# Grouping the products of probabilities and values three by three in the TensorE order of a clustered attention kernel

## The chip, the cores and the metric

The kernel runs on one core of one Trainium2 chip. The metric is the device time of one execution in microseconds (us), as the median of three runs.

## What is computed

The kernel computes three layers. First comes attention in which each query sees only the keys of its own cluster (2 batches, 8 heads, 768 positions, 64 columns each, 16 clusters):

```
mask = q_assign[:, :, :, None] == k_assign[:, :, None, :]
scores = scale * np.matmul(q, k.transpose(0, 1, 3, 2))
scores = np.where(mask, scores, -1000000000.0)
scores = scores - np.max(scores, axis=-1, keepdims=True)
attn = np.exp(scores)
attn = attn / (np.sum(attn, axis=-1, keepdims=True) + 1e-09)
return np.matmul(attn, v).astype(np.float32)
```

Here `q_assign` and `k_assign` are the nearest of 16 centroids by cosine. Its output, as 1536 tokens of 512 columns, goes through a layer of 8 experts of which each token takes one (512 to 1024 to 512 columns), and that output through a gated layer, `(x @ w_a) * (x @ w_b) @ w_out`, with 1536 inner columns. Only the attention is touched by the change.

## The kernel before, in words

The 16 pairs of batch and head are called heads here. The attention is a software pipeline over rounds `r`: in round `r` TensorE works on four heads at once. Each engine has one instruction queue, worked strictly in the order in which the program wrote it, with semaphores between the engines; nothing reorders it. The order of TensorE's queue is written out by hand in the loop over `rounds[2:]` (from line 1260 on), one line for each step:

- `scores_t(r, j)`, six times (lines 1212 and 1214): the transposed scores of key tile `j` of head `r`, 128 keys by 768 queries in two halves. ScalarE turns them into probabilities (`exps`, line 601). There are three PSUM banks for these halves.
- `times_v(r, j)`, six times (line 1227): the product of the probabilities of key tile `j` with its values, four recorded matmuls for the two halves of the queries, added up in the bank `o_ps` over the six tiles. It waits for the exponentials of its tile; the first waits also until the sum of the head before has been taken out of the bank, and the last releases `o_full`.
- `masked_scores(n, t)`, six times, for head `n = r + 2` (line 1174): the masked scores of query tile `t`, in one pair of banks, `pair`. VectorE takes each row's maximum out of it (`row_max`, `neg_max`, line 863). There is one such pair, so tile `t` waits for the maximum of tile `t - 1` (`mx_done`).
- `unit0(n, 0)` to `unit0(n, 6)` for head `n = r + 3`: transposes of queries and keys (units 0 to 3, line 1144), products with the centroids (units 4 and 5, line 1148) and a transpose of the logits (unit 6, line 1152), and units 7 and 8 (lines 1157 and 1160) for head `r + 2`. They share one bank `t0`: every unit waits until the one before it was taken out by ScalarE or VectorE. Unit 0 waits for `has_key` (line 907), which frees the bank after unit 8 of the head before.
- `unit1(kind, n)`: `max` for head `r + 1`, and `sum`, `out`, `mean` for head `r - 1`. They share the bank `t1`. `sum` (line 1188) adds the probabilities of head `r - 1` over the keys; `out` (lines 1194 and 1195) turns the attention output and the denominators `den` of head `r - 1` and waits until VectorE has made `den` (line 834).

VectorE's order around this is: after unit 8 it makes `has_key` (907), `has_tmp` (909), `found` (913) and `lost` (914), then `den` (834), then one copy of unit 1, the maxima of tiles 0 to 2, the copies of `high_parts` (795 and 797, for head `r + 4`), the maxima of tiles 3 and 4, `one_hot` (873 to 880), and the maximum of tile 5.

GpSimd adds up the probabilities (`add_probs`, line 346): the add of tile 1 waits for `sum` of head `r - 1`, the add of tile 2 follows directly, and the adds of tiles 3, 4 and 5 come later in the round, with `fill_lost` and `low_parts` between them. In the last two rounds VectorE does these adds.

Round 0 has no `sum`, `out` and `mean`, and takes in the masked scores of head 1 between its steps. Rounds 13 to 15 have no units 0 to 6, rounds 14 and 15 no masked scores either; these two have transposes for the next layer (`turn_x`, line 1241) instead. Where `out` is named below as a place, its first matmul (line 1194) is meant.

Of the kernel before, what the change touches and what calls it, by code (L numbers as in the profile page):

```python
# [73 lines left out]
def build(nc, q, k, v, centroids, expert_emb, tau, w1, w2, w_a, w_b, w_out, consts, out):  # L74
# [5 lines left out]
    with whole:  # L80
# [221 lines left out]
        def made(r):  # L302
            return {-3: [0, 1], -2: [2], -1: []}.get(r, [r + 3] if 0 <= r < HEADS - 3 else [])

        def masked(r):
            return {-2: [0, 1], -1: []}.get(r, [r + 2] if 0 <= r < HEADS - 2 else [])
# [19 lines left out]
        def early_tile(r, place):  # L326
            return [NT - 3 * (HEADS - r) + place] if HEADS - 2 <= r < HEADS else []
# [9 lines left out]
        def valid(n):  # L337
            return 0 <= n < HEADS
# [780 lines left out]
        def _(pe):  # L1119
# [44 lines left out]
            def masked_scores(n, t):  # L1164
                u = n % 4
                if t == 0:
                    pe.wait_ge(ops_in[u], 64 * (n // 4 + 1))
                two = masked_in(n, t)
                if n == 0 and t >= 2:
                    pe.wait_ge(mx_done, t - 1)  # L1170
                elif n > 0:
                    pe.wait_ge(mx_done, 6 * n + t)
                for half in range(2):
                    last = pe.matmul(two[:, half, 0:HALF], qb[u][0:96, t * P:(t + 1) * P],  # L1174
                                     kc[u][0:96, half * HALF:(half + 1) * HALF], start=True, stop=True)
                last.then_inc(mx_full, 1)

            def unit1(kind, n):
                i = t1_index[kind, n]
                if i:  # L1180
                    pe.wait_ge(t1_free, i)
                if kind == "max":
                    pe.wait_ge(mx_done, 6 * n + 6)
                    last = pe.transpose(t1[0:NT, 0:P], neg_max[n % 2][:], ident)
                elif kind == "sum":
                    pe.wait_ge(psum_ready, n + 1)
                    for half in range(2):
                        last = pe.matmul(t1[half * 32:half * 32 + 32, 0:HALF], ones_f[:, 0:32],
                                         prob_sum[:, half * HALF:(half + 1) * HALF], start=True, stop=True)
                elif kind == "out":  # L1190
                    pe.wait_ge(o_taken, n + 1)
                    pe.wait_ge(t1_free, t1_index["sum", n] + 1)
                    for j in range(3):
                        pe.transpose(t1[:, j * P:(j + 1) * P], o_sb[:, j * P:(j + 1) * P], ident)
                        last = pe.transpose(t1[:, HALF + j * 33:HALF + (j + 1) * 33], den[0:33, j * P:(j + 1) * P],
                                            cst[0:33, 0:33])
                else:
                    pe.wait_ge(vsum_ready, n + 1)
                    last = pe.matmul(t1[:, 0:D], ones_f[:], v_sum[n % 2][:], start=True, stop=True)
                last.then_inc(t1_full, 1)  # L1200

            def scores_t(n, j):

                u = n % 4
                if j == 0:
                    pe.wait_ge(max_in[u], 16 * (n // 4 + 1))
                for half in range(2):
                    i = 12 * n + 2 * j + half
                    if i >= 3:
                        pe.wait_ge(exp_done, i - 2)  # L1210
                    cols = slice(half * HALF, (half + 1) * HALF)
                    pe.matmul(st[i % 3][:, 0:HALF], kd[u][:, j * P:(j + 1) * P], qa[u][:, cols],  # L1212
                              start=True, stop=False)
                    pe.matmul(st[i % 3][:, 0:HALF], kc[u][0:97, j * P:(j + 1) * P], qb[u][0:97, cols],  # L1214
                              start=False, stop=True).then_inc(st_full, 1)

            def times_v(n, j):
                u, s = n % 4, n % 2
                pe.wait_ge(exp_done, 12 * n + 2 * j + 2)
                if j == 0:  # L1220
                    pe.wait_ge(v_in[u], 16 * (n // 4 + 1))
                    if n == 0:
                        pe.wait_ge(second_free, 9)
                    if n >= 1:
                        pe.wait_ge(o_taken, n)
                for half in range(2):
                    last = pe.matmul(o_ps[half * D:(half + 1) * D, 0:HALF], v_in_sb[u][:, j, :],  # L1227
                                     prob[s][:, j, half * HALF:(half + 1) * HALF],
                                     start=(j == 0), stop=(j == NT - 1))
                if j == NT - 1:  # L1230
                    last.then_inc(o_full, 1)

            def turn_x(j, to):

                if j == 0:
                    pe.wait_ge(x_done, H)
                    pe.wait_ge(mx_done, 6 * HEADS)
                if j >= 2:
                    pe.wait_ge(xt_taken, j - 1)
                for kk in range(KD):  # L1240
                    last = pe.transpose(to[:, kk * P:(kk + 1) * P], x_tok[:, j, kk * P:(kk + 1) * P], ident)
                last.then_inc(xt_full, 1)

            def logits(c):

                pe.wait_ge(xt_taken, max(3 * c + 3, 5 if c == 0 else 0))
                if c == 3:
                    pe.wait_ge(o_taken, HEADS)
                for kk in range(KD):
                    last = pe.matmul(logits_in[c][0:E, 0:HALF], en_t[:, kk, :],  # L1250
                                     x_t[c // 2][:, kk, (c % 2) * HALF:(c % 2 + 1) * HALF],
                                     start=(kk == 0), stop=(kk == KD - 1))
                last.then_inc(lgt_full, 1)

            for r in rounds[2:]:
                s_, p4 = valid(r), valid(r - 1)
                if s_: scores_t(r, 0)
                if r == 0: masked_scores(1, 2)
                for n in masked(r)[:1]: unit0(n, 7)
                if s_: scores_t(r, 1)  # L1260
                if r == 0: masked_scores(1, 3)
                if valid(r + 1) and r != 0: unit1("max", r + 1)
                if r == -1:
                    masked_scores(1, 0)
                    masked_scores(1, 1)
                if s_: scores_t(r, 2)
                if r == 0: masked_scores(1, 4)
                if p4: unit1("sum", r - 1)
                for n in masked(r)[:1]: unit0(n, 8)
                if s_: times_v(r, 0)  # L1270
                for n in made(r): unit0(n, 0)
                if r == 0: masked_scores(1, 5)
                if s_: times_v(r, 1)
                for t in early_tile(r, 0): turn_x(t, pair[:, t % 2, :])
                for n in made(r): unit0(n, 1)
                for n in masked(r)[:1]: masked_scores(n, 0)
                if r == -2: unit0(1, 7)
                if p4: unit1("out", r - 1)
                if r == HEADS: logits(0)
                for n in made(r): unit0(n, 2)  # L1280
                if s_: scores_t(r, 3)
                for n in masked(r)[:1]: masked_scores(n, 1)
                if r == -2: unit0(1, 8)
                for t in early_tile(r, 1): turn_x(t, pair[:, t % 2, :])
                for n in made(r): unit0(n, 3)
                if p4: unit1("mean", r - 1)
                if r == HEADS: logits(1)
                if s_: scores_t(r, 4)
                for n in masked(r)[:1]: masked_scores(n, 2)
                if r == -3: centroids_turned()  # L1290
                for n in made(r): unit0(n, 4)
                if s_: times_v(r, 2)
                if r == 0: unit1("max", 1)
                for n in masked(r)[:1]: masked_scores(n, 3)
                for n in made(r): unit0(n, 5)
                if s_: times_v(r, 3)
                for n in masked(r)[:1]: masked_scores(n, 4)
                if s_: scores_t(r, 5)
                for n in made(r): unit0(n, 6)
                if s_: times_v(r, 4)  # L1300
                for t in early_tile(r, 2): turn_x(t, pair[:, t % 2, :])
                for n in masked(r)[:1]: masked_scores(n, 5)
                if s_: times_v(r, 5)


            pe.wait_ge(x_done, HEADS)
# [193 lines left out]
```

## Time and profile before

| | |
|---|---|
| time before, median of 3 runs | 1043.55 us (1041.11 to 1053.14) |
| span of the profiled execution | 1031.7 us |
| TensorE busy | 888.3 us, 86% of the span |
| VectorE busy | 540.5 us, 52% |
| ScalarE busy | 293.2 us, 28% |
| GpSimd busy | 345.1 us, 33% |
| mean granted clock of TensorE | 0.932 |

The profile is of one execution; it records each instruction with its start, its duration, its engine and the program's line, and what ended the idle time before it. The span goes from the first to the last instruction; the device time of a run holds some 12 us more. The granted clock is given as a share of 2.4 GHz: 1.00 is 2.4 GHz, 0.50 is 1.2 GHz.

### The profile page before, as it was taken

To read this page: it belongs to the slowest core of one execution; us is meant where nothing else is said; L and a number is where in the kernel's file an instruction comes from. 1 tells how busy PE (TensorE), PEld (TensorE's weight loads), DVE (VectorE), ACT (ScalarE), POOL (GpSimd) and SP (SyncE) were. 2 spreads that over 40 slices of the span, in tenths; PEclk is the share of its full clock that TensorE was granted. 3 is DMA by queue.
4 is the path that set the end of the run, shared out by engine and by line. 5 is a ranking of instruction groups with operands and counts; after the bars stand their busy time and mean duration, and the time that the engine had idled before them with its cause. 6 is when DMAs were issued, how large, how long until landed. Compare 5 with 4: busy or idle time off the path is not lost.

```text
span 1031.7 us, 11850 instructions
## 1 busy us (share of the span) xinstructions
PE 888.3 (86%) x4205; PEld 626.6 (61%) x4206; DVE 540.5 (52%) x663; ACT 293.2 (28%) x558; POOL 345.1 (33%) x195
## 2 busy tenths in 40 slices
PE   5899999899999994287897778876999999999998
PEld 2545555555555542165675566764888888888886
DVE  5678788887787647156644664462621321131111
ACT  3234333343333334032331233131321211121111
POOL 5145665556554423634412442142500100000000
PEclk9599999999899897599999999887999999999999
DMA  4212322223211204554245523552100200000001
GB/s 116 71 46 76 86 83 71 64 74 88 63 45 50 102 27 173 214 193 176 95 147 193 189 97 132 194 193 82 62 1 1 62 21 1 1 29 13 1 1 41
DMA packets 41105, 86.93 MB, mean 84 GB/s; under 512 B 4216, under 2 KB 10584, under 8 KB 41056
## 3 DMA queue, kind: packets, MB, share of 16 engines
q1 hardware_dynamic: 39136, 79.99, 23.7%
q0 software_dynamic: 1920, 6.29, 1.8%
q8 instruction: 30, 0.49, 0.2%
q14 instruction: 19, 0.16, 0.0%
HBM read 60.53 MB, written 17.83 MB: 76 GB/s over the span
## 4 chain that ended last, share of the span: by engine, by line
PE 68%; DVE 15%; issue 13%; ACT 2%; DMA 1%; DVEq 1%; ACTq 0%; SPq 0%; POOL 0%
PE bank L1427 7%; PE bank L1428 7%; PE bank L1429 7%; PE bank L1227 4%; PE pair L1174 4%; PE first_pair L1212 3%; DVE wt L978 3%; PE bank L1367 3%; PE bank L1369 2%; PE first_pair L1214 2%; PE bank L1368 2%; DVE has_tmp L909 2%; PE bank L1212 2%; PE bank L1144 2%; PE first_pair L1444 2%
## 5 line engine op out<-in xcount | busy, mean ns | idle before, releaser
L552 POOL TENSOR_TENSOR wt<-w_raw,wt 128x2048 fp32r<-128x2048 f32 x20 | 118.3, 5935 | 180.3 <-DVE wt L970 180.2
L1101 DVE TENSOR_TENSOR g_sb<-bank,a_sb 128x512 f32<-128x512 f32 x36 | 24.9, 691 | 195.0 <-PE bank L1429 195.0
L978 DVE TENSOR_TENSOR wt<-w_raw,wt 128x2048 fp32r<-128x2048 f32 x21 | 116.3, 5543 | 2.0 <-ACT wt L680 1.8
L1427 PE MATMUL bank<-x_hi,wt 128*128 128x512 f32 x288 | 114.9, 399 | 1.4 <-DVE x_lo L1072 1.4
L1428 PE MATMUL bank<-x_lo,wt 128*128 128x512 f32 x288 | 114.5, 398 | 0.0
L1429 PE MATMUL bank<-x_hi,wt 128*128 128x512 f32 x288 | 114.5, 398 | 0.0
L863 DVE TENSOR_REDUCE neg_max<-pair 128x1 f32<-128x768 f32 x93 | 88.5, 951 | 43.8 <-PE pair L1174 43.8
L346 POOL TENSOR_TENSOR prob_sum<-prob_sum,prob 128x768 f32<-128x768 f32 x56 | 102.5, 1831 | 10.4 <-ACT prob L601 8.4
L1367 PE MATMUL bank<-wt,ht_hi 128*128 128x512 f32 x128 | 59.0, 461 | 50.0 <-DVE ht_lo L1042 50.0
L601 ACT ACTIVATE prob<-first_pair 128x384 f32<-128x384 f32 x128 | 59.5, 486 | 83.8 <-PE first_pair L1214 51.6
L1227 PE MATMUL bank<-prob,v_sb 128*64 128x384 f32 x384 | 82.7, 514 | 0.0
L1174 PE MATMUL pair<-kc,qb 96*128 96x384 f32 x186 | 60.1, 408 | 6.5 <-DVE neg_max L863 5.9
L1427 PEld LDWEIGHTS bank<-x_hi,wt 128*128 128x128 f32 x288 | 54.6, 190 | 15.1 <-DVE x_lo L1072 1.8
L1042 DVE TENSOR_TENSOR ht_lo<-bank,ht_hi 128x512 fp32r<-128x512 f32 x32 | 21.9, 684 | 79.5 <-ACT ht_hi L705 79.5
L1429 PEld LDWEIGHTS bank<-x_hi,wt 128*128 128x128 f32 x288 | 54.5, 189 | 13.4
L1367 PEld LDWEIGHTS bank<-wt,ht_hi 128*128 128x128 f32 x128 | 26.3, 206 | 59.8 <-DVE ht_lo L1042 34.1
L1428 PEld LDWEIGHTS bank<-x_lo,wt 128*128 128x128 f32 x288 | 54.6, 190 | 13.2
L761 ACT ACTIVATE a_sb<-bank 128x512 f32<-128x512 f32 x36 | 21.5, 598 | 129.8 <-PE bank L1429 129.7
L1174 PEld LDWEIGHTS pair<-kc,qb 96*128 96x128 f32 x186 | 33.6, 213 | 36.7 <-DVE neg_max L863 25.9
L1358 PE MATMUL first_pair<-wt,xt_hi 128*128 128x512 f32 x128 | 53.6, 419 | 1.9 <-DVE xt_lo L1036 1.9
L1368 PE MATMUL bank<-wt,ht_hi 128*128 128x512 f32 x128 | 55.0, 430 | 0.0
L1369 PE MATMUL bank<-wt,ht_lo 128*128 128x512 f32 x128 | 55.0, 430 | 0.0
(213 smaller groups left out, 1752.3 us busy)
## 6 DMA issues: line engine op xcount, KB each, us to landing
w_raw<-in_moe_w_dram SPq DMA_DIRECT2D x32, 1024.0 KB, 5.8
x_slots<-zeros SPq DMA_DIRECT2D x10, 512.0 KB, 3.6
x_slot<-x_slots SPq DMA_DIRECT2D x18, 256.0 KB, 3.0
y_slots<-y_sb SPq DMA_DIRECT2D x16, 256.0 KB, 2.3
q_raw<-in_q_dram SPq DMA_DIRECT2D x16, 192.0 KB, 2.4
k_raw<-in_k_dram SPq DMA_DIRECT2D x16, 192.0 KB, 2.5
v_sb<-in_v_dram SPq DMA_DIRECT2D x16, 192.0 KB, 2.4
qb<-qa SPq DMA_DIRECT2D x16, 192.0 KB, 2.6
```

The source lines that it names most:

```text
L346: ins = eng.tensor_tensor(prob_sum[:], prob[s][:, 0, :] if j == 1 else prob_sum[:], prob[s][:, j, :], ALU.add)
L552: pool.tensor_tensor(wt[chunk][:, 1, :], w_raw[c][:], wt[chunk][:, 0, :].bitcast(F32), ALU.subtract).then_inc(w_lo[1], 1)
L863: dve.tensor_reduce(neg_max[n % 2][:, t:t + 1], masked_in(n, t)[:, :, 0:HALF], AX.XY, ALU.max, negate=True).then_inc(mx_done, 1)
L978: dve.tensor_tensor(wt[chunk][:, 1, :], w_raw[c][:], wt[chunk][:, 0, :].bitcast(F32), ALU.subtract).then_inc(w_lo[0], 1)
L1174: last = pe.matmul(two[:, half, 0:HALF], qb[u][0:96, t * P:(t + 1) * P], kc[u][0:96, half * HALF:(half + 1) * HALF], start=True, stop=True)
L1227: last = pe.matmul(o_ps[half * D:(half + 1) * D, 0:HALF], v_in_sb[u][:, j, :], prob[s][:, j, half * HALF:(half + 1) * HALF], start=(j == 0 ...
L1367: pe.matmul(bank[5][:, :], ht_hi[:, ff, :], w[0], start=(ff == 0), stop=False)
L1368: pe.matmul(bank[5][:, :], ht_hi[:, ff, :], w[1], start=False, stop=False)
L1369: last = pe.matmul(bank[5][:, :], ht_lo[:, ff, :], w[0], start=False, stop=(ff == FT - 1))
L1427: pe.matmul(to[:, :], w[0], x2_hi[:, kk, :], start=(kk == 0), stop=False)
L1428: pe.matmul(to[:, :], w[0], x2_lo[:, kk, :], start=False, stop=False)
L1429: last = pe.matmul(to[:, :], w[1], x2_hi[:, kk, :], start=False, stop=(kk == KD - 1))
```

## The change

Four of the six `times_v` of a round are moved in TensorE's order, so that tiles 0, 1 and 2 stand directly behind one another at the place where tile 2 stood (behind `unit0(n, 4)`), and tiles 3, 4 and 5 at the place where tile 5 stood, at the end of the round. No instruction is added or removed, and no other engine's order is touched.

```diff
@@ -1267,10 +1267,8 @@
                 if r == 0: masked_scores(1, 4)
                 if p4: unit1("sum", r - 1)
                 for n in masked(r)[:1]: unit0(n, 8)
-                if s_: times_v(r, 0)
                 for n in made(r): unit0(n, 0)
                 if r == 0: masked_scores(1, 5)
-                if s_: times_v(r, 1)
                 for t in early_tile(r, 0): turn_x(t, pair[:, t % 2, :])
                 for n in made(r): unit0(n, 1)
                 for n in masked(r)[:1]: masked_scores(n, 0)
@@ -1289,18 +1287,18 @@
                 for n in masked(r)[:1]: masked_scores(n, 2)
                 if r == -3: centroids_turned()
                 for n in made(r): unit0(n, 4)
-                if s_: times_v(r, 2)
+                if s_:
+                    for j in (0, 1, 2): times_v(r, j)
                 if r == 0: unit1("max", 1)
                 for n in masked(r)[:1]: masked_scores(n, 3)
                 for n in made(r): unit0(n, 5)
-                if s_: times_v(r, 3)
                 for n in masked(r)[:1]: masked_scores(n, 4)
                 if s_: scores_t(r, 5)
                 for n in made(r): unit0(n, 6)
-                if s_: times_v(r, 4)
                 for t in early_tile(r, 2): turn_x(t, pair[:, t % 2, :])
                 for n in masked(r)[:1]: masked_scores(n, 5)
-                if s_: times_v(r, 5)
+                if s_:
+                    for j in (3, 4, 5): times_v(r, j)
```

## Rows read from the trace of the kernel before

**Rows 1.** TensorE's waits in the attention: us in total, times, longest.
```profile
PE bank L1194 <- DVE den L834: 18.3, 14, 2.0
PE pair L1174 <- DVE neg_max L863: 4.0, 9, 0.6
```

**Rows 2.** TensorE's timeline, head 8, up to `out`: start us, duration us, instruction.
```profile
221.93 0.87 PE L1227 MATMUL bank<-prob,v_sb 128*64 128x384 f32 x4
222.72 0.55 PE L1144 MATMUL bank<-cst,q_split 128*128 128x128 f32 x3
223.20 0.87 PE L1227 MATMUL bank<-prob,v_sb 128*64 128x384 f32 x4
224.00 0.55 PE L1144 MATMUL bank<-cst,q_split 128*128 128x128 f32 x3
226.25 0.30 PE L1194 MATMUL bank<-cst,o_sb 128*128 128x128 f32 x1 [1.35 <-DVE den L834]
```

**Rows 3.** The timeline of GpSimd and VectorE in the same stretch.
```profile
221.91 1.82 POOL L346 TENSOR_TENSOR prob_sum<-prob 128x768 f32<-128x768 f32 x1 [3.54 <-PE bank L1188]
222.24 1.55 DVE L909 TENSOR_TENSOR has_tmp<-hot,has_key 128x96 bf16<-128x96 bf16 x1
223.81 1.81 POOL L346 TENSOR_TENSOR prob_sum<-prob_sum,prob 128x768 f32<-128x768 f32 x1
224.11 1.53 DVE L914 TENSOR_SCALAR lost<-found 128x6 f32<-128x6 f32 x1
225.56 0.54 DVE L834 TENSOR_SCALAR den<-bank 33x384 f32<-33x384 f32 x1
```

**Rows 4.** The tile `has_tmp`: duration ns min/median/max over all heads.
```profile
L909 DVE TENSOR_TENSOR has_tmp<-hot,has_key x16: 207/1548/1551, 26.8 to 333.8; 128x96 bf16<-128x96 bf16 x16
```

**Rows 5.** TensorE's timeline, head 8, from the third product to the next head.
```profile
231.48 0.87 PE L1227 MATMUL bank<-prob,v_sb 128*64 128x384 f32 x4
...
234.95 0.62 PE L1174 MATMUL pair<-kc,qb 96*128 96x384 f32 x2 [0.50 <-DVE neg_max L863]
235.41 0.34 PE L1212 MATMUL first_pair<-qa,kd 128*128 128x384 f32 x1
...
236.21 0.57 PE L1152 MATMUL bank<-cst,logit_sb 48*128 48x48 f32 x6
236.71 0.87 PE L1227 MATMUL bank<-prob,v_sb 128*64 128x384 f32 x4
237.50 0.62 PE L1174 MATMUL pair<-kc,qb 96*128 96x384 f32 x2
...
238.85 0.45 PE L1212 MATMUL first_pair<-qa,kd 128*128 128x384 f32 x1
```

**Rows 6.** VectorE's timeline in that stretch: a cast, the maximum of tile 4.
```profile
232.06 1.97 DVE L797 CAST k_split<-k_raw 128x384 fp32r<-128x384 f32 x1
...
235.61 0.96 DVE L863 TENSOR_REDUCE neg_max<-pair 128x1 f32<-128x768 f32 x1 [0.71 <-PE pair L1174]
```

**Rows 7.** TensorE's timeline, round 13: two products in a row, masked scores, `out`.
```profile
333.46 1.51 PE L1227 MATMUL bank<-prob,v_sb 128*64 128x384 f32 x8
335.19 0.62 PE L1174 MATMUL pair<-kc,qb 96*128 96x384 f32 x2 [0.22 <-DMA kc<-hot_t]
337.76 0.30 PE L1194 MATMUL bank<-cst,o_sb 128*128 128x128 f32 x1 [1.96 <-DVE den L834]
```

**Rows 8.** Windows: us, TensorE busy (instructions), granted clock, DMA share, GB/s.
```profile
71.48:333.46 261.98, 241.24 (x1336) 0.95 0.25 68
200.76:221.93 21.17, 19.24 (x115) 1.00 0.28 77
265.20:288.74 23.54, 22.09 (x114) 0.85 0.20 53
185.00:188.20 3.20, 3.20 (x14) 0.51 0.09 20
338.60:345.30 6.70, 6.70 (x22) 0.50 0.00 0
```

## The prediction, made before the kernel ran

> **What bounds the kernel.** TensorE is busy for 86% of the span, so I read its waits first. The reader is to see in them that a full TensorE queue does not make its order free: 14 times in the attention `out` waits for `den`, 18.3 us together, far more than the 4.0 us for row maxima [rows 1]. So I read one full head (round 8; the twelve rounds 1 to 12 have this pattern) on all engines, then the grouped products that the trace already has, and last the clock by head.
>
> Between the end of unit 8 (221.93) and `out` (226.25) lie 4.32 us. TensorE fills them with two products, units 0 and 1 and a masked score, and idles 1.35 us [rows 2]. What lasts 4.32 us is VectorE's chain `has_key`, `has_tmp`, `found`, `lost`, `den`. Two of its small operations are long for what they do: `has_tmp` takes 1.55 us from 222.24 and ends with GpSimd's add at 223.7, `lost` takes 1.53 us and ends with the second add at 225.6 [rows 3]. Where no add ran, `has_tmp` took 0.207 us [rows 4]. The first add is released by `sum`, which stands ahead of the moved products. Nothing in this chain hangs on products 0 and 1, so it will not get shorter when they leave.
>
> The Trainium skill (SBUF: State Buffer, section "SBUF: two separate sides") says why: VectorE and GpSimd share a port pair as an exclusive lock, and the later one blocks for the whole instruction. The trace agrees with 1.55 against 0.207 us. This speaks against the change, since it makes the place of `den` independent of how TensorE is filled.
>
> **Part 1: products 0 and 1 leave the cover.** They take 0.79 (221.93 to 222.72) and 0.80 us (223.20 to 224.00) [rows 2], 1.6 us a head that were free under VectorE's chain. They are now paid later, and the idle time ahead of `out` grows from 1.35 to about 2.95 us. Part of that will be seen earlier: unit 0 reaches its wait for `has_key`, and unit 1 its wait for ScalarE's copy of unit 0. Neither moves `out`, nor does the masked score's wait for the DMA of `hot_t`: round 13, which has no units 0 and 1, waits 0.22 us for it and then another 1.96 us for `den`, and its `out` starts 4.30 us after unit 8, as in the full head [rows 7].
>
> **Part 2: grouping.** Alone, a product costs 0.80 us. Two behind each other are recorded with 1.51 us, one with 0.87 [rows 2, 7], so a second or third one costs 0.64. A group of three is 0.80 + 2 x 0.64 = 2.08 us, and a head saves 4 x 0.16 = 0.64 us.
>
> **Part 3: from the third product to the next head.** Now this takes 238.85 - 231.48 = 7.37 us, and it holds 0.50 us of waiting for the maximum of tile 3 [rows 5]. That wait has VectorE's cast in front (1.97 us, 232.06 to 234.03) [rows 6]. After the change the group of three comes before masked score 3, so the cast is over; but then unit 5 alone stands between masked scores 3 and 4. The turn from one masked score to the next cannot be shorter than 0.66 (234.95 to 235.61) + 0.96 for the maximum + some 0.04 of signalling = 1.66 us [rows 5, 6]. The new stretch:
>
> group 2.08; masked score 3 to 4, 1.66; masked score 4, 0.46 (to 235.41); scores 0.80 (to 236.21); unit 6, 0.50 (to 236.71); masked score 5, 0.55 (237.50 to 238.85, less a product of 0.80); group 2.08. Sum 8.13 us, against 7.37: +0.76 a head [rows 5].
>
> Masked score 5 doesn't wait: 0.46 + 0.80 + 0.50 = 1.76 is over 1.66. Unit 7 of the next head needs `hot`; the last group gives it 2.08 us against 0.80 now, so no loss there. `o_full` and so the loads of values and the exponentials' buffers come at the same place, at the end of the round. SP's queue sees nothing new.
>
> By rounds: 1 to 11, 11 x 0.76 = 8.4. Round 12 has no cast, so its 0.50 us wait doesn't exist today: +0.76 + 0.50 = 1.3. Round 0 likewise +1.3, less about 0.3, because products 0 and 1 stand among waits for other engines there: 1.0. Round 13 has neither unit 5 nor unit 6 as cover: 2.08 + 1.66 + 1.66 + 0.55 + 2.08 = 8.03 after; today's parts at full clock are four products 3.2, three masked scores 1.6, scores 0.8 and some 0.25 of waiting, 5.85: +2.2. Rounds 14 and 15 have pairs today; each saves 2 x 0.16: -0.6. Sum: 8.4 + 1.3 + 1.0 + 2.2 - 0.6 = **+12.3 us at an unchanged clock**. Its bounds: the hand-over from the small transposes to a product may save up to another 0.2 us a head, so 9; if waits show up that I take as hidden (0.2 us a head), 15.
>
> **Part 4: the clock.** A head takes 21.17 us at a clock of 1.00, but the twelve heads from 71.48 to 333.46 take 261.98 us, 7.9 us more than 12 x 21.17 [rows 8]. Six of the twelve have a stretch at 0.50 (1.2 GHz), and so has round 13; each begins shortly behind the wait for `den`, in round 13 at 338.60, 0.84 us after `out` started [rows 7, 8]. Five of the six are as short as the one of 3.20 us shown; the sixth is about twice as long and makes its head 23.54 us, 2.4 more than a full one, so the other five cost (7.9 - 2.4)/5 = 1.1 us each [rows 8]. Round 13, whose waits ahead of `out` are the longest (0.22 + 1.96) [rows 7], has 6.70 us at 0.50 [rows 8]. After the change every one of 13 heads has such a gap, 2.95 us instead of 1.35. I expect a slow stretch in all of them. A short one costs 1.1 now where the 0.50 us wait of part 3 swallows some; that wait is gone, so 1.6. 13 x 1.6 = 20.8 us, less what is paid now, 7.9 + 2.4 = 10.3: **+10 us**. Bounds: nothing, if the falls stay as rare; 13 x 2.4 - 10.3 = +21, if all are long.
>
> [...]
>
> **The sum.** 12.3 + 10 = 22.3 us on the profiled span of 1031.7: 1054. The median of the runs is 1043.55, 11.9 above that span, so 1043.55 + 22.3 = 1065.9, said as **1066 us**.
>
> **Rivals.**
> - *No more slow stretches.* The idle time ahead of `out` is now split in three, with units 0 and 1 between, and the clock may hold as often as now. Then 1043.6 + 12.3 = 1056 us (1052 to 1059). Against it: round 13's long slow stretch.
> - *All slow stretches long.* For it: round 13 again. 1043.6 + 12.3 + 21 = 1077 us.
> - *Faster.* One mechanism: `den` comes earlier. If GpSimd's adds no longer fell together with `has_tmp` and `lost`, each would give back 1.55 - 0.21 = 1.34 us [rows 3, 4], 2.7 a head, all of it idle time now uncovered. It decides from 0.76 us a head on. With both gone, the 12 full heads come out at 0.76 - 2.68 = -1.9 us each, 23 in all, and with the rest of the sum and fewer slow stretches 1017 us. Against it: `sum` releases the first add and unit 8 releases `has_key`, and both keep their places.
> - *About even.* One of the two collisions goes: 0.76 - 1.34 = -0.6 us a head, 7 in all, which the other rounds (+2.2, +1.0, +1.3) and some slow stretches make up: 1044 us.
>
> **How the numbers follow.** Forecast 0.55, no more slow stretches 0.22, all long 0.11, about even 0.07, faster 0.05. The range 1051 to 1080 takes in the forecast and both neighbours; what is left out is even and faster (0.12) and some tail. A measurement of this kernel can tell about 1% from no change: 1054 is slower. Forecast, all long and 0.16 of the first rival lie above: slower 0.82, same 0.13, faster 0.05.
>
> **What would show it.** In the changed kernel's profile: two groups of twelve recorded matmuls of line 1227 in each head, 2.1 us each; `has_tmp` and `lost` still 1.5 us, and `out` still 4.3 us after unit 8; the waits of units 0 and 1 and of `out` together near 3 us a head; a wait for `neg_max` near 0.4 us ahead of masked score 4, and two in round 13; heads of 21.9 us at a clock of 1.00 and some 23 us with a slow stretch. The prediction is wrong if the chain to `den` gets shorter, if a third product in a row costs 0.8, or if the clock falls no more often than in seven of thirteen heads.

## The result, and the profile after

The changed kernel takes 1068.62 us (median of 4 runs, 1067.29 to 1072.57). The kernel before, beside it, had 1042.33 us (1032.97 to 1053.14). The ratio is 1.032, with a 95% interval of 1.026 to 1.038: slower.

In the later comparisons the kernel before has medians of 1035 to 1037 us over 51 runs on three chips, between 1029 and 1046; the three runs that the prediction started from were on the high side. The changed kernel, run again beside it, has 1069.06 against 1035.3 us, a ratio of 1.033 (1.026 to 1.041). So the step is 26 to 34 us, by which of the two pairs one takes, where 22 were forecast.

TensorE's waits in the attention of the changed kernel (us in total, times, longest), to be read beside [rows 1]:

```profile
PE bank L1194 <- DVE den L834: 24.6, 15, 2.0
PE bank L1144 <- ACT qa L613: 7.0, 12, 0.6
PE pair L1174 <- DVE neg_max L863: 5.2, 15, 1.0
PE bank L1144 <- DVE has_key L907: 3.2, 12, 0.3
PE pair L1174 <- DMA kc<-hot_t: 2.1, 3, 1.6
```

The wait for `den` has grown, and two waits are there that [rows 1] does not have: unit 1 for ScalarE's copy of unit 0 (twelve times 0.58 us) and unit 0 for `has_key` (twelve times 0.27). One full head on TensorE's timeline (start, duration, instruction, and in brackets the idle time before it and what ended it; `...` marks instructions left out):

```profile
228.20 2.16 PE L1227 MATMUL bank<-prob,v_sb 128*64 128x384 f32 x12
...
231.95 0.62 PE L1174 MATMUL pair<-kc,qb 96*128 96x384 f32 x2 [0.29 <-DVE neg_max L863]
...
233.71 0.62 PE L1174 MATMUL pair<-kc,qb 96*128 96x384 f32 x2
234.26 2.16 PE L1227 MATMUL bank<-prob,v_sb 128*64 128x384 f32 x12
236.34 0.44 PE L1212 MATMUL first_pair<-qa,kd 128*128 128x384 f32 x1
...
240.22 0.31 PE L1160 MATMUL bank<-hot,ones_bf 128*128 128x16 bf16 x6
240.80 0.55 PE L1144 MATMUL bank<-cst,q_split 128*128 128x128 f32 x3 [0.27 <-DVE has_key L907]
241.92 0.55 PE L1144 MATMUL bank<-cst,q_split 128*128 128x128 f32 x3 [0.58 <-ACT qa L613]
242.22 0.59 PE L1174 MATMUL pair<-kc,qb 96*128 96x384 f32 x2
244.76 0.45 PE L1194 MATMUL bank<-cst,o_sb 128*128 128x128 f32 x1 [1.95 <-DVE den L834]
```

The reader is to see three things. First, from the start of the first group to the next head it is 236.34 - 228.20 = 8.14 us, where [rows 5] have 7.37 from the third product on. Second, the waits ahead of `out` are 0.27 + 0.58 + 1.95 = 2.80 us, where [rows 2] have 1.35. Third, `out` starts 3.98 us after `has_tmp` (240.78 in the rows below to 244.76), where it was 4.01 (222.24 to 226.25) [rows 2, 3]. VectorE in the same stretch, beside [rows 3]:

```profile
240.78 1.54 DVE L909 TENSOR_TENSOR has_tmp<-hot,has_key 128x96 bf16<-128x96 bf16 x1
242.35 0.25 DVE L913 TENSOR_REDUCE found<-has_tmp 128x6 f32<-128x96 bf16 x1
242.64 1.52 DVE L914 TENSOR_SCALAR lost<-found 128x6 f32<-128x6 f32 x1
244.08 0.54 DVE L834 TENSOR_SCALAR den<-bank 33x384 f32<-33x384 f32 x1
```

From `has_tmp` to the start of `den` it is 3.30 us, where it was 3.32, so the chain is unchanged. Last the windows (us, TensorE busy, granted clock, DMA share, GB/s), first the twelve heads of rounds 1 to 12, then two single ones, then a part of the second of these from `out` on:

```profile
72.86:360.03 287.17, 250.65 (x1334) 0.88 0.23 62
216.89:240.22 23.33, 20.23 (x113) 0.93 0.26 71
240.22:264.42 24.20, 21.11 (x113) 0.86 0.24 67
244.76:250.00 5.24, 5.24 (x19) 0.50 0.17 38
```

The twelve heads took 261.98 us in [rows 8]; now it is 25.2 us more. No head is left at a clock of 1.00: nine of the twelve take 24.0 to 24.3 us at 0.86, three take 23.3 at 0.93. In the head shown the granted clock has fallen to half (1.2 GHz) when `out` starts, as the last row shows.

### The profile page after: what moved, and what is told of

It reads as the page before. It is cut to its first block, busy times and chain, and to the rows that moved or that the text cites. A ratio compares the mean times of both kernels' runs of the same rounds, so it can differ in the third digit from the quotient of the medians.

```text
span 1065.9 us, 11850 instructions
## 1 busy us (share of the span) xinstructions
PE 909.9 (85%) x4205; PEld 654.7 (61%) x4206; DVE 547.6 (51%) x663; ACT 294.9 (28%) x558; POOL 343.8 (32%) x195
## 4 chain that ended last, share of the span: by engine, by line
PE 70%; DVE 13%; issue 12%; ACT 2%; DMA 1%; DVEq 1%; SPq 0%; ACTq 0%; POOL 0%
PE bank L1425 6%; PE bank L1227 6%; PE bank L1426 6%; PE bank L1427 6%; PE pair L1174 4%; PE first_pair L1212 3%; PE bank L1365 3%; DVE wt L978 3%; PE bank L1367 2%; PE bank L1366 2%; PE first_pair L1214 2%; DVE has_tmp L909 2%; PE bank L1144 2%; DVE neg_max L863 2%; PE bank L1212 2%
## 5 line engine op out<-in xcount | busy, mean ns | idle before, releaser
L1365 PE MATMUL bank<-wt,ht_hi 128*128 128x512 f32 x128 | 63.4, 495 | 43.2 <-DVE ht_lo L1042 43.2
L1227 PE MATMUL bank<-prob,v_sb 128*64 128x384 f32 x384 | 70.7, 504 | 0.0
L1365 PEld LDWEIGHTS bank<-wt,ht_hi 128*128 128x128 f32 x128 | 29.4, 229 | 54.2 <-DVE ht_lo L1042 28.0
L1366 PE MATMUL bank<-wt,ht_hi 128*128 128x512 f32 x128 | 59.0, 461 | 0.0
L1367 PE MATMUL bank<-wt,ht_lo 128*128 128x512 f32 x128 | 58.8, 460 | 0.0
```

What stands on the lines that cost most here:

```text
L1365: pe.matmul(bank[5][:, :], ht_hi[:, ff, :], w[0], start=(ff == 0), stop=False)
L1366: pe.matmul(bank[5][:, :], ht_hi[:, ff, :], w[1], start=False, stop=False)
L1367: last = pe.matmul(bank[5][:, :], ht_lo[:, ff, :], w[0], start=False, stop=(ff == FT - 1))
```

## The experiments

Each was compared with the kernel before on the same chip. "Heads" are the rounds 1 to 12, each from the start of unit 8 to that of the next. The runs are called e1 to e12; each indented text is what was expected of one before it ran. Ratios are to the kernel before, with their 95% interval.

### One group without the other

The first run, e1, groups products 0 to 2 alone:

```diff
-                if s_: times_v(r, 0)
...
-                if s_: times_v(r, 1)
...
-                if s_: times_v(r, 2)
+                if s_:
+                    for j in (0, 1, 2): times_v(r, j)
```

> Only products 0, 1 and 2 are grouped at the place of product 2; products 3, 4 and 5 stand where they stood before. My theory: the whole cost comes from products 0 and 1 leaving the stretch in which TensorE waits for den. The gap ahead of out is that of the changed kernel (some 2.9 us in three parts), slow-clock stretches in every head as there. From the third product's place to the next head: group 2.08, masked score 3 with unit 5 and product 3 behind it 2.10 (over the 1.66 that the row maximum needs, so no wait), 0.46, 0.80, 0.50, 0.80, 0.55, 0.80 = 8.09 us against 8.13 in the changed kernel. Time within 3 us of the changed kernel, 1064 to 1070 us. Rival (both groups cost alike, by the waits that they open between masked scores): half of the loss, about 1055 us.

Measured: 1062.92 us, ratio 1.027 (1.018 to 1.037). Heads of 24.0 to 24.6 or 23.3 us, the twelve together 287.53 us:

```profile
74.30:361.83 287.53, 253.81 (x1334) 0.88 0.23 62
```

That is the 287.17 us of the changed kernel. The first group alone makes the whole loss in the heads. The median is 1 us under the range expected and 6 under the changed kernel's; the interval (1055.5 to 1074.7 us) holds the latter and just not the rival's 1055. The expected 8.09 us from the third product's place to the next head came as 8.08 (278.23 to 286.31).

The second, e2, groups products 3 to 5 alone:

```diff
-                if s_: times_v(r, 3)
...
-                if s_: times_v(r, 4)
...
-                if s_: times_v(r, 5)
+                if s_:
+                    for j in (3, 4, 5): times_v(r, j)
```

> Only products 3, 4 and 5 are grouped at the end of the round; 0, 1 and 2 stand where they stood before. My theory: the gap ahead of out stays at 1.35 us and the clock falls as often as in the kernel before. Product 3 no longer covers the wait for the maximum of tile 3, so that wait grows from 0.50 to 1.30 us, and the group saves 0.32: heads of 21.17 + 0.49 = 21.66 us at full clock. Rounds 1 to 11 cost 5.4 us, round 13 some 0.9: about +6 us, 1046 to 1052 us. Rival (both groups cost alike): about 1055 us.

Measured: 1047.17 us, ratio 1.011 (1.006 to 1.017). The one head at full clock, and in a later head the wait for the maximum of tile 3:

```profile
71.56:93.12 21.56, 18.91 (x114) 1.00 0.28 76
```
```profile
128.91 0.61 PE L1174 MATMUL pair<-kc,qb 96*128 96x384 f32 x2 [1.30 <-DVE neg_max L863]
```

The wait is 1.30 us, as expected, and a head 21.56 us (21.66 expected, 21.17 before). But the clock did not fall "as often as before": only this first head stayed at 1.00, and the twelve took 276.81 us, 18 more than 12 x 21.56. Three of the falls begin about 2 us behind this wait, which is 1.30, 1.13 and 0.98 us there (in the head of the row shown at 130.8, 1.9 us after it). I had not foreseen that this wait could do it. The others begin around `out`, which waits 1.35 us as in the kernel before but has a fall around it in ten heads instead of six; why is open. So the time lies in the range expected in part by luck: that range was counted from the high start of 1043.55, and beside its partner of 1036.82 the step is 10 us, where 6 were expected. This part costs something too where the gap ahead of `out` is short; beside the first group it adds nothing to the heads (e1 against the changed kernel).

### The gap filled

In e3 the changed kernel gets small matmuls ahead of `out`:

```diff
+            def keep_busy(r, count):
+                pe.wait_ge(o_taken, r)
+                for i in range(count):
+                    pe.matmul(o_ps[:, HALF:512], ident, ident, start=True, stop=True, skip_group_check=True)
...
+                if p4 and masked(r): keep_busy(r, 8)
                 if p4: unit1("out", r - 1)
```

> The changed kernel with eight small matmuls (128 by 128, their result is not used by anyone) put ahead of out in rounds 1 to 13, where TensorE waits for den, so that it is busy there instead of idle. Nothing is left out of the computation. My theory: 12 full heads of 24.15 or 23.33 us hold 24 us of loss by the clock's fall behind the gap. With the gap filled the falls go, heads take 21.93 us at a clock of 1.00, out still starts 4.3 us after unit 8, and the time is 1040 to 1048 us. Rival (the clock falls for another reason, or the small matmuls only push out later): no gain, 1066 us or more.

Measured: 1039.99 us, ratio 1.003 (1.000 to 1.007), at the lower edge of what was expected. The twelve heads, one of them, and TensorE ahead of `out` (the eight small matmuls are recorded as 16):

```profile
77.00:338.81 261.81, 246.16 (x1527) 1.00 0.25 69
229.75:251.58 21.83, 20.52 (x130) 1.00 0.27 75
```
```profile
232.18 1.95 PE L1258 MATMUL bank<-cst 128*128 128x128 f32 x16
234.30 0.30 PE L1194 MATMUL bank<-cst,o_sb 128*128 128x128 f32 x1 [0.17 <-DVE den L834]
```

With useless work in the gap the kernel is 29 us faster than without (1069.06 us in e8; 3.0% by the two ratios to the kernel before), and all twelve heads run at 1.00. A head takes 21.82 us, and `out` starts where it did. This shows the clock term on its own: 287.17 - 261.81 = 25.4 us in the twelve heads.

> The kernel before with five of the same small matmuls ahead of out, in its idle 1.35 us. Nothing is left out. My theory: heads of 21.17 us at full clock and no falls behind out; 8 to 18 us less than the kernel before, 1024 to 1036 us. The difference to the changed kernel with its gap filled is then what the order costs at an unchanged clock, forecast at 12.3 us. Rival (matmuls of this size don't hold the clock): 1040 to 1046 us.

This run is e4. The edit was e3's, with `keep_busy(r, 5)` on the kernel before. But there products 0 and 1 stand ahead of `keep_busy`, and their sum in the same bank is still open; the small matmuls, though they write other columns, spoiled it. So the attention's sum is not the reference's, the experts get other tokens, and the 1040.44 us (ratio 1.004) say nothing. The attention's timing can be read: twelve heads in 253.43 us at 1.00, 21.17 each without the last, shorter one.

> The kernel before with five small matmuls ahead of out in rounds 1 to 13, their unused result in the spare columns of a score bank that is free there; in e4 they stood in the bank in which products 0 and 1 were still being added up, and spoiled that sum, so e4 is of use for the attention's timing alone. Nothing is left out. My theory: heads of 21.17 us at a clock of 1.00 as in e4, 8 to 15 us less than the kernel before on the same chip, and about 11 us less than e3. Rival (the time before, 1037 us, holds little loss by falls of the clock): within 3 us of the kernel before.

In this run, e5, the same matmuls go to `st[0][:, HALF:512]`, behind a wait for `exp_done` at `12 * r + 6`. Measured: 1024.82 us, ratio 0.990 (0.983 to 0.997).

```profile
70.97:324.37 253.40, 244.15 (x1455) 1.00 0.26 71
```

Rounds 1 to 12 take 253.40 us, where they took 261.98 [rows 8]: 8.6 us less in the heads, and 10.5 in all. The 8 to 15 expected held. e3 minus e5 is 261.81 - 253.40 = 8.4 us in these rounds: eleven heads of 21.82 against 21.17, and round 12 with 21.80 against 20.54. The whole difference is larger than the 11 us expected, 16.9 us between the two spans: 6.0 up to round 1, 8.4, -1.1 in rounds 13 to 15, where e5 has a slow stretch, and 3.6 in the layers behind, whose cause is open (see the sum below).

### The chain to `den` shortened

This edit, with most of the sum of probabilities left out, is made on the kernel before (e6) and on the changed one (e7):

```diff
-            ins = eng.tensor_tensor(prob_sum[:], prob[s][:, 0, :] if j == 1 else prob_sum[:],
-                                    prob[s][:, j, :], ALU.add)
+            w = slice(0, 8) if 1 <= n < DVE_ADDS and j in (1, 2) else slice(0, S)
+            ins = eng.tensor_tensor(prob_sum[:, w], prob[s][:, 0, w] if j == 1 else prob_sum[:, w],
+                                    prob[s][:, j, w], ALU.add)
```

> The kernel before, with GpSimd's adds of key tiles 0 to 2 cut from 768 columns to 8 for heads 1 to 13, so most of their sum of probabilities is left out; only the attention's timing is read. My theory: has_tmp and lost fall to 0.2 us each, den is ready 2.7 us sooner, out no longer waits for it and starts right behind the masked score, 2.95 us after unit 8 instead of 4.32. Heads of about 19.8 us at full clock. Rival (the two are slow for another reason than GpSimd's adds): out stays at 4.3 us.

> The changed kernel with the same cut. My theory: with den ready before TensorE comes, products 0 and 1 were under no cover to begin with, so moving them costs nearly nothing: out starts 2.3 to 2.5 us after unit 8, heads are 19.8 to 20.1 us at full clock, within 0.3 us of e6, where the uncut pair differs by 0.66 (21.82 against 21.17). Slow-clock stretches become rare again. Rival (the cost is the masked scores' turn at the end of the round): heads 0.66 us longer than those of e6 or more.

Timeline and one head of e6. The edit adds a line to the program, so lines 909, 914 and 1194 are 910, 915 and 1195 here:

```profile
211.50 0.22 DVE L910 TENSOR_TENSOR has_tmp<-hot,has_key 128x96 bf16<-128x96 bf16 x1
212.04 0.17 DVE L915 TENSOR_SCALAR lost<-found 128x6 f32<-128x6 f32 x1
214.00 0.27 PE L1195 MATMUL bank<-cst,o_sb 128*128 128x128 f32 x1
```
```profile
92.70:112.33 19.63, 19.03 (x113) 1.00 0.31 83
```

e7, one head:

```profile
195.55:215.25 19.70, 18.56 (x113) 1.00 0.31 83
```

`has_tmp` falls from 1.55 to 0.22 us and `lost` from 1.53 to 0.17; `out` starts without a wait. Now the change costs 0.07 us a head at full clock, where it cost 0.65 with the chain as it is (21.82 in e3, 21.17 before). In e7 two of the twelve heads hold a slow stretch instead of all. There is one execution of each, but the heads repeat: ten of e6 lie at 19.6 and seven of e7 at 19.7 (e7's first three at 19.9 to 20.1).

The whole times are 1004.45 us for e6 and 1017.50 for e7, still 13 us apart. Of this 4.7 us lie in the twelve heads, by the two slow stretches, the first three heads and the 0.07 each, 3.9 in round 0, which is 23.47 us in e7 with a slow stretch at its start and 19.55 in e6, and 4.9 behind the twelve heads (the start is 0.4 shorter). So the short chain takes away the loss in a full head, and not every cost of the change.

The Trainium skill (SBUF — State Buffer, "SBUF: two separate sides") has the shared port pair as an exclusive lock for the whole instruction; these runs agree, with 1.33 and 1.36 us less for the two once the adds are short.

> The changed kernel itself, beside the others on the same chip, so that e1 and e3 have their partner. It should give a ratio of about 1.03 to the kernel before, heads of 24.15 us with a long slow-clock stretch or 23.33 with a short one, and none without.

Measured in this run, e8: 1069.06 us, ratio 1.033 (1.026 to 1.041). Heads of 24.0 to 24.4 or 23.3 us, none at 1.00.

### `den` ahead of the long operations

VectorE's order is changed on the kernel before (e9) and on the changed one (e10):

```diff
+                if p4: denominators(r - 1)
                 for n in masked(r)[:1]: find_keys(n)
...
-                if p4: denominators(r - 1)
```

> The kernel before with one change in VectorE's order: den is made ahead of has_key, has_tmp, found and lost instead of behind them. My theory (what binds is VectorE's chain to den, of which only den's place matters): out starts right behind the masked score, 2.9 us after unit 8 instead of 4.3, and does not wait. The copy of unit 1 still stands behind lost, so unit 2 starts about 1.3 us earlier, not more. Heads of 19.9 us at full clock, falls of the clock rare: 1010 to 1024 us. Rival (the copy of unit 1 or the cast takes den's place as the bound): heads within 0.3 us of 21.17, about 1030 us.

> The changed kernel with the same edit of VectorE's order. My theory: out starts 2.5 us after unit 8, but unit 2 then waits for the copy of unit 1, which still stands behind lost, so the cover for products 0 and 1 is still needed and still missing. Heads of 20.5 us at full clock, 0.6 above e9; the gap is cut to 1.5 us in pieces, so slow-clock stretches get fewer but stay more frequent than in e9: 1022 to 1045 us. Rival (den's place was all): within 5 us of e9.

Measured: e9 1011.02 us, ratio 0.974 (0.968 to 0.980); e10 1028.64 us, ratio 0.991 (0.988 to 0.994). One head of each, at full clock:

```profile
210.95:230.84 19.89, 19.16 (x114) 1.00 0.30 82
```
```profile
198.10:218.67 20.57, 18.70 (x113) 1.00 0.29 79
```

Both came as expected (19.9 and 20.5). e9 computes all that the reference does and beats both kernels by 2.6% and more; none of its twelve heads has a slow stretch. e10 shows that the place of `den` was not all: unit 2 then waits for the copy of unit 1, which still stands behind `lost`:

```profile
202.56 0.55 PE L1144 MATMUL bank<-cst,k_split 128*128 128x128 f32 x3 [0.47 <-DVE qa L843]
```

TensorE still needs products 0 and 1 as cover there, so the change keeps costing 0.68 us a head, and three of the twelve heads have slow stretches where e9 has none. No single wait around `out` is longer than 0.6 us there.

### The same grouping in another place

In e11, beside the kernel before:

```diff
-                if s_: times_v(r, 0)
+                if s_:
+                    for j in (0, 1, 2): times_v(r, j)
...
-                if s_: times_v(r, 1)
...
-                if s_: times_v(r, 2)
...
-                if s_: times_v(r, 3)
+                if s_:
+                    for j in (3, 4): times_v(r, j)
...
-                if s_: times_v(r, 4)
```

> The kernel before with products 0, 1 and 2 grouped where product 0 stood, ahead of the wait for den, products 3 and 4 grouped where 3 stood, and 5 in its place. Same grouping in threes for the first three, other place. My theory: not the grouping but the place costs. The three products (2.08 us) lie in the 4.3 us of VectorE's chain, the gap ahead of out shrinks to some 0.5 us, and the clock falls less often. Heads of 20.8 to 21.2 us at full clock, since the cast and one_hot on VectorE hold the second half. 1022 to 1034 us, 35 us or more under the changed kernel. Rival (products in a row are bad in themselves): 1045 us or more.

Measured: 1033.57 us, ratio 0.999 (0.996 to 1.001). The group of three costs the same 2.16 recorded us, but lies under VectorE's chain, and `out` waits 0.20 us:

```profile
223.79 2.16 PE L1227 MATMUL bank<-prob,v_sb 128*64 128x384 f32 x12
...
228.10 0.30 PE L1194 MATMUL bank<-cst,o_sb 128*128 128x128 f32 x1 [0.20 <-DVE den L834]
...
241.78 0.49 PE L1157 MATMUL bank<-ident_bf,hot 128*32 128x128 bf16 x6 [0.87 <-DVE hot L880]
```

So a group of three is not bad in itself: placed here it is some 35 us (3.5% by the ratios) better than in the change. Nor does it gain at full clock (21.15 us a head), because unit 7 of the next head then waits 0.87 us for `hot`. Four of the twelve heads have a slow stretch, short ones, though `out` waits only 0.2 us. In the first of these heads unit 1 waits 0.58 us and `out` 0.19, and the clock falls at 121.0, 1.5 us after `out` starts:

```profile
118.36 0.55 PE L1144 MATMUL bank<-cst,q_split 128*128 128x128 f32 x3 [0.58 <-ACT qa L613]
...
119.45 0.30 PE L1194 MATMUL bank<-cst,o_sb 128*128 128x128 f32 x1 [0.19 <-DVE den L834]
```
```profile
121.00:124.30 3.30, 3.30 (x15) 0.51 0.27 60
```

So with a shorter wait ahead of `out` there are fewer falls, four of twelve where the kernel before has six, but they don't end.

The last run, e12, is e9 with this one edit more:

```diff
-                if s_: times_v(r, 3)
+                if s_:
+                    for j in (3, 4): times_v(r, j)
...
-                if s_: times_v(r, 4)
```

> e9 with product 4 moved up behind product 3, into the wait for the maximum of tile 3. Theory: it fills 0.5 us of waiting, so 0.1 to 0.6 us a head are gained unless one_hot's last operation, held by GpSimd's last add, binds unit 7 of the next head: 2 to 7 us under e9. Rival (one_hot binds): within 2 us of e9.

Measured: 1012.01 us, ratio 0.976 (0.970 to 0.982), the same as e9 within what these runs can tell. TensorE's waits in the attention:

```profile
PE bank L1157 <- DVE hot L880: 11.2, 13, 0.9
PE pair L1174 <- DVE neg_max L863: 0.6, 2, 0.3
```

The wait for the maximum of tile 3 is gone (6.7 us in e9), and the wait for `hot` has come in its place. The rival was right.

## Why the prediction was right, point by point

**Part 1, products 0 and 1 leave the cover: right.** `out` starts 4.54 us after the start of unit 8 (240.22 to 244.76), where it was 4.56; the forecast's 4.3 counts from its end. The moved 1.6 us are paid, and the waits ahead of `out` are 2.80 us (2.95 expected). e1 shows that this group alone makes the loss in the heads, e6 and e7 that a head's loss at full clock nearly vanishes with the chain's length: 0.07 us instead of 0.65.

**Part 2, grouping: right.** A group is recorded with 2.16 us, which is the 0.87 of one and 2 x 0.645.

**Part 3, the second half: right.** 8.14 us against 8.13. The turn from masked score 3 to 4 takes 231.95 - 230.29 = 1.66 us. In round 13 the two turns have waits of 1.05 and 0.35 us, as that round's sum supposes. A whole head costs 0.65 us more and not 0.76: unit 7 now finds `hot` ready, and gains the 0.1 us that I had put down as "no loss". Eleven heads cost 7.2 us, where 8.4 were forecast, and round 12 1.27, where 1.3 were. Rounds 13 to 15 at full clock, from unit 8 to the last `out`: 46.9 us in e3 and 44.3 in e4, +2.6 against +1.6. That makes 11.1 us at an unchanged clock, without round 0, of which no pair of runs shows both at full clock; the forecast without it was 11.3.

**Part 4, the clock: the mechanism right, the size too small.** A slow stretch in every one of 13 heads was forecast and came. The term put down 1.6 us for each and so +10 us. Measured in the twelve heads: 287.17 - 261.81 = 25.4 us, 2.1 a head, against 261.98 - 253.40 = 8.6 in the profile before, so +17. Nine of twelve stretches are long ones, which cost 2.3 us, three are short ones of 1.5. The short one was sized well; that most would be long was the rival with 0.11. Round 13, whose waits ahead of `out` were the most like those to come, had shown a long one, and I gave it too little weight. This mis-sized term is the main reason that the step came out larger than forecast.

**Round 0: missed.** Forecast +1.0 us, measured 22.69 - 19.56 = +3.1 from unit 8 to unit 8. With products 0 and 1 gone, unit 0 waits 1.70 us for `has_key` there, where it was 0.88, and a slow stretch of 6.8 us begins 0.4 us behind that wait; [rows 8] begin behind this round, and I had looked for falls of the clock only behind `out`.

**The sum.** The spans differ by 1065.9 - 1031.7 = 34.2 us: the start -1.5, round 0 +3.1, the twelve heads +25.2, rounds 13 to 15 +3.9, the two layers behind +3.5. Forecast 22.3. The layers behind were put at nothing; behind the last `out` they take 651.9 us before and 655.4 after, but in the other kernels' profiles anything from 649.9 (e2) to 656.4 (e9), so it is not shown that their +3.5 comes from the change. The absolute time, 1066 forecast and 1068.6 measured, is closer than the step, and that is partly luck: the starting median of 1043.55 was 7 us above what the kernel before showed in most later runs. That some 12 us of a run's time lie around the profiled span was wrong too. In the changed kernel it is 1.8 us (1067.68 against 1065.9); the profile before was of a faster execution than those of the median.

## What to carry to other kernels

In a queue that is worked in order, independent work is worth what it covers: before moving it, find which chain on another engine ends during it, and what in that chain depends on the moved work. Price the waits that open not only by their length but also by the clock: here 2.80 us of waits ahead of `out` brought a slow stretch in every head and cost up to 2.3 us more behind them. Shorter waits are not safe: with 1.35 us six of twelve heads had a slow stretch, and with 0.58 and 0.2 us (e11) four had. And before filling a wait, look at what stands ahead of its releaser in its queue: moving one 0.54 us operation ahead of two that another engine holds up gained 2.6% (2.0 to 3.2), more than any order of TensorE's work tried here.

## What the runs showed of the hardware that I had not expected

- Work of no use can pay: small matmuls ahead of `out`, whose result nobody reads, took 29 us off the changed kernel and 1.0% off the kernel before. TensorE's granted clock then stayed at 2.4 GHz through all twelve heads.
- A fall of the clock needs no long idle: in the kernel before it came behind waits of 1.35 us followed by small transposes, in e2 also behind waits of 0.98 to 1.30 us, and in e11 behind waits of 0.58 and 0.2 us. Yet half the heads with the same 1.35 us had none, so the length of a wait alone does not settle it here. The Trainium skill (TensorE: Matmul & The Clock Gate, Part 1) shows falls by longer waits, against which the measurement decides; in the same part it also describes a kernel in which frequent short idle times between groups of matmuls made the clock swing, and that is nearer to what these traces show.
- Matmuls that start a sum of their own in spare columns of a bank where another sum is open spoil that sum (e4); in another bank (e5), or in the same bank with no sum open (e3), they don't. The Trainium skill (PSUM — Partial Sum Buffer, "The four PSUM rules") says that the first matmul of a sum clears the "has been written" marks of the whole bank for each group of 32 partitions it writes, so that the next matmul of the open sum overwrites instead of adding; the three runs agree with that.
